# A fused attention, expert and MLP kernel: token rows in a DRAM region per expert, scattered in three rounds, and 32 idle matmuls between the loads of the branch codes

## Chip, cores and metric

The kernel runs on one core of one Trainium2 chip. The metric is the device time of one execution in microseconds (us), taken as the median of the runs. A profiled execution gives the trace; its times are counted from the start of its span.

## The reference, cut to what matters

Three layers in a row on 2 x 768 tokens of 384 values: a decayed linear attention, a layer that sends each token to one of eight experts, and a dense MLP with two matrices. The part that the change is about:

```python
x = attn_out.transpose(0, 2, 1, 3).reshape(B * S, H * D)      # token index = batch * 768 + position
logits = x @ w_gate                                           # 1536 x 8
expert_idx = np.argmax(logits, axis=1)
probs = softmax(logits); gate_w = probs[np.arange(N), expert_idx]
for i in range(N):                                            # the first `capacity` (384) tokens of an expert
    e = expert_idx[i]
    if counts[e] < capacity:
        disp[e, counts[e]] = x[i]; pos[i] = counts[e]; counts[e] += 1; keep[i] = True
y = np.einsum('ecf,efd->ecd', np.maximum(np.einsum('ecd,edf->ecf', disp, w1), 0.0), w2)
out[i] = gate_w[i] * y[expert_idx[i], pos[i]] if keep[i] else 0
h = out @ w_in
out = (np.maximum(h, 0) + alpha * np.minimum(h, 0)) @ w_out
```

## The kernel before, in words

Every f32 operand of the expert and MLP matmuls is split into a high and a low part (type fp32r), and a product is three matmuls: high x high, high x low, low x high (lines 1150 to 1152), or two where both parts of h are streamed at once (1160, 1161). ScalarE writes high parts, VectorE low parts.

The attention runs in three frames of 256 positions, each in eight steps of TensorE (`attend`, s = 2 to 9): transposes of q and k of a group, scores of the one before, and the product with v and the state of the one before that (`apply_group`, 1001). State tiles w0, w1, w2 are kept on VectorE's side; w0 starts as zeros and is first rewritten in `shift_state` (736 to 739) at step 8 of frame 0. A token tile has 128 tokens; there are twelve, by block of positions and batch. In the last frame the gate is worked in between: `x_transpose` (1041) turns a tile, ScalarE evicts it (483), `tile_logits` (1049) multiplies by w_gate; `LOGITS_AT` says which tiles go to which step.

After the last logits VectorE works on all twelve tiles at once (821 to 865): largest logit, one_hot of the chosen expert, gate weight. TensorE counts tokens per tile and expert (1128) and ranks them (1129 to 1133), so that VectorE gets one slot per token (`slots_i`), with the experts' tokens in one dense list of 1536. It raises `routed`, and then writes `base_i`: for each expert the first slot, plus 4096 (WIDE) if it has over 224 tokens (NARROW). GpSimd then issues twelve indirect scatters (369), which write each token's row of 388 values (384, gate weight and token number, two unused) to the DRAM tensor `rows_by_slot`. When all have landed, SyncE loads the list back as twelve tiles (308). TensorE turns each with three transposes of 128 x 128 (1144), ScalarE and VectorE write xs_hi and xs_lo (551, 877), which hold all 1536 tokens. Expert 0 starts when its tiles are there; `wait_ge(row_lo, rows)` asks for three tiles for expert 0 and for all twelve from expert 1 on.

An expert reads 224 columns of xs from its first slot (or 384 in the other branch), and has eight chunks of weights. Per chunk, `hidden(i)` makes 128 rows of h with nine matmuls, ScalarE and VectorE split h (561, 886), and `output(i)` adds to three PSUM banks with six matmuls. TensorE runs hidden two chunks ahead of output. Weights come by DMA from SyncE into a ring of eight buffers; ScalarE (543) and VectorE (870) split each six chunks ahead. The splits of chunks 0 to 5 stand ahead of the row tiles on both engines. TensorE reads the eight codes from base_i into registers (`value_load`, which the order of instructions shows as TENSOR_LOAD) before the transposes; ScalarE and VectorE read one ahead of each expert. In the profiled execution every expert took the branch of 224.

The order on each engine is the one written in the code; engines meet in semaphores only.

## Time and profile before

| | us |
|---|---|
| median of 3 runs (lowest, highest) | 549.45 (549.38, 549.66) |
| profiled execution | 548.02 |
| its span | 546.10 |
| TensorE matmuls busy | 467.5 (86%) |
| VectorE busy | 363.7 (67%) |
| ScalarE busy | 272.3 (50%) |
| GpSimd busy | 42.9 (8%) |
| mean granted clock of TensorE | 0.952 of full |

Busy time counts the engine's instructions, without register, branch and semaphore instructions. The granted clock is the share of full speed that TensorE was given; 0.50 is 1.2 GHz and 1.00 is 2.4 GHz. TensorE's load of weights has rows of its own (PEld) and runs beside the matmuls. A chain of waits names, from the end back, what each step waited for.

### The profile page before, as it was taken

Reading aid. Unit: us, or ns where it says so; the run is one execution under the profiler, and the core shown is the slowest. Engines: PE = TensorE matmul, PEld = TensorE weight load, DVE = VectorE, ACT = ScalarE, POOL = GpSimd, SP = SyncE. Lnnn points to the kernel's source line nnn. Section 1 sums busy time; section 2 is a strip of 40 time slices with the busy share of each in tenths; the row PEclk is TensorE's granted clock in tenths of the full one; section 3 lists DMA queues with packets and bytes.
Section 4 is the critical chain, followed back from the end, with each engine's and each line's share of the span. In section 5 each row is a group of like instructions: output and inputs, shape, how many; then the busy total and the mean of one; then the engine's idle time right before and its main releaser. Section 6 shows DMA issues by size and latency. Waiting matters only on the chain.

```text
span 546.1 us, 10002 instructions
## 1 busy us (share of the span) xinstructions
PE 467.5 (86%) x3752; PEld 417.7 (76%) x3752; DVE 363.7 (67%) x624; ACT 272.3 (50%) x431; POOL 42.9 (8%) x48
## 2 busy tenths in 40 slices
PE   0538976999996029999999999999999999999995
PEld 0237755777885029999999998989998899889985
DVE  2688798678534317776777776778747787487751
ACT  5996758673446017666666664433334333334212
POOL 2000000000001890000000000000002000110002
PEclk9959999999998559999999999999999999999999
DMA  8970000000000469667666666233324333230001
GB/s 323 424 294 2 3 1 1 2 1 2 2 3 2 159 188 324 182 192 215 205 195 199 200 189 190 89 99 104 96 78 145 102 101 114 70 108 0 1 0 60
DMA packets 22178, 63.69 MB, mean 117 GB/s; under 512 B 2928, under 2 KB 4464, under 8 KB 22128
## 3 DMA queue, kind: packets, MB, share of 16 engines
q1 hardware_dynamic: 20592, 58.27, 32.6%
q0 software_dynamic: 1536, 4.74, 2.3%
q8 instruction: 32, 0.52, 0.4%
q14 instruction: 18, 0.15, 0.1%
HBM read 58.27 MB, written 4.74 MB: 115 GB/s over the span
## 4 chain that ended last, share of the span: by engine, by line
PE 74%; DVE 8%; DMA 5%; issue 5%; POOL 3%; ACT 2%; SPq 2%; DVEq 0%; POOLq 0%; ACTq 0%
PE banks L1152 15%; PE banks L1150 15%; PE banks L1151 15%; PE banks L1160 7%; DMA vv<-v_rows 4%; PE banks L1161 3%; PE banks L998 3%; POOL rows_by_slot L369 3%; PE banks L986 2%; PE banks L1017 2%; PE banks L989 2%; PE banks L950 2%; PE banks L1020 1%; PE banks L1144 1%; PE banks L1046 1%
## 5 line engine op out<-in xcount | busy, mean ns | idle before, releaser
L870 DVE TENSOR_TENSOR w_lo<-raw_early,w_hi 128x768 fp32r<-128x768 f32 x84 | 80.0, 956 | 31.1 <-ACT w_hi L543 30.0
L588 ACT ACTIVATE g_hi<-g_all 128x512 fp32r<-128x512 f32 x48 | 30.3, 632 | 118.4 <-DVE g_all L923 118.4
L543 ACT ACTIVATE w_hi<-raw_early 128x768 fp32r<-128x768 f32 x84 | 70.4, 843 | 33.2 <-PE banks L1161 32.7
L1150 PE MATMUL banks<-w_hi,g_hi 128*128 128x384 f32 x192 | 65.1, 339 | 0.5 <-DVE g_lo L925 0.5
L1152 PE MATMUL banks<-w_hi,g_lo 128*128 128x384 f32 x192 | 65.0, 339 | 0.0
L1151 PE MATMUL banks<-w_lo,g_hi 128*128 128x384 f32 x192 | 64.9, 338 | 0.0
L1160 PE MATMUL banks<-h_hi_lo,w_hi 128*128 128x448 f32 x192 | 64.0, 378 | 0.9 <-DVE h_hi_lo L886 0.9
L925 DVE TENSOR_TENSOR g_lo<-g_all,g_hi 128x512 fp32r<-128x512 f32 x48 | 33.3, 693 | 44.2 <-ACT g_hi L588 44.2
L1150 PE MATMUL banks<-ys_hi,w_hi 128*128 128x512 f32 x144 | 56.1, 390 | 1.2 <-DVE ys_lo L900 1.2
L1152 PE MATMUL banks<-ys_hi,w_lo 128*128 128x512 f32 x144 | 57.1, 397 | 0.0
L1151 PE MATMUL banks<-ys_lo,w_hi 128*128 128x512 f32 x144 | 56.8, 394 | 0.0
L1150 PE MATMUL banks<-xs_hi,w_hi 128*128 x192 | 52.7, 274 | 0.1
L1151 PE MATMUL banks<-xs_lo,w_hi 128*128 x192 | 52.6, 274 | 0.0
L1152 PE MATMUL banks<-xs_hi,w_lo 128*128 x192 | 52.6, 274 | 0.0
L1161 PE MATMUL banks<-h_hi_lo,w_lo 128*128 128x224 f32 x192 | 50.9, 265 | 0.0
L921 DVE TENSOR_SCALAR g_neg<-banks,alpha 128x512 f32<-128x512 f32 x48 | 35.8, 746 | 7.5 <-PE banks L1152 7.4
L1160 PEld LDWEIGHTS banks<-h_hi_lo,w_hi 128*128 128x128 f32 x192 | 36.2, 189 | 4.4 <-DVE h_hi_lo L886 2.1
L1150 PEld LDWEIGHTS banks<-w_hi,g_hi 128*128 128x128 f32 x192 | 36.1, 188 | 3.4 <-DVE g_lo L925 1.5
L1151 PEld LDWEIGHTS banks<-w_lo,g_hi 128*128 128x128 f32 x192 | 36.1, 188 | 2.1
L1150 PEld LDWEIGHTS banks<-xs_hi,w_hi 128*128 128x128 f32 x192 | 36.7, 191 | 1.1 <-issue 0.4
L377 POOL DMA_INDIRECT out_rows<-xq,tok_slot x12 | 11.9, 991 | 324.5 <-ACT xq L597 322.7
L1152 PEld LDWEIGHTS banks<-xs_hi,w_lo 128*128 128x128 f32 x192 | 36.9, 192 | 0.0
(166 smaller groups left out, 981.2 us busy)
## 6 DMA issues: line engine op xcount, KB each, us to landing
raw_early<-weights SPq DMA_DIRECT2D x84, 384.0 KB, 3.5
raw_late<-weights SPq DMA_DIRECT2D x28, 384.0 KB, 3.5
xq<-q_rows SPq DMA_DIRECT2D x3, 776.0 KB, 16.6
xq<-rows_by_slot SPq DMA_DIRECT2D x12, 194.0 KB, 4.5
kk<-k_rows SPq DMA_DIRECT2D x3, 768.0 KB, 18.0
vv<-v_rows SPq DMA_DIRECT2D x3, 768.0 KB, 19.4
aa<-a_re_rows SPq DMA_DIRECT2D x2, 768.0 KB, 10.5
th<-a_im_rows SPq DMA_DIRECT2D x2, 768.0 KB, 11.9
```

What stands on the lines that cost most here:

```text
L369: pool.indirect_dma_start(xs_dram, bass.IndirectOffsetOnAxis(ap=slots_i[:, t:t + 1], axis=0), xq[:, x:x + XW], None).then_inc(scattered, 16)
L543: A(wh[:, slot, :], raw[slot], ACT.Copy).then_inc(w_hi, 1)
L588: A(gh[:, c % GBUF, :], gg[:, c % GBUF, :], ACT.Copy).then_inc(g_hi, 1)
L870: TT(wl[:, slot, :], raw[slot], wh[:, slot, :].bitcast(F32), ALU.subtract).then_inc(w_lo, 1)
L921: TS(gn[:, :], HM[c % HBUF][:, :], 0.0, alpha[:, i:i + 1], ALU.min, ALU.mult).then_inc(g_neg, 1)
L925: TT(gl[:, c % GBUF, :], gg[:, c % GBUF, :], gh[:, c % GBUF, :].bitcast(F32), ALU.subtract).then_inc(g_lo, 1)
L998: x = MM(SC[g % 2][:, c], lhsT=kT[:, g % 2, c], rhs=qT[:, g % 4, c], start=True, stop=True)
L1150: MM(o, lhsT=whi, rhs=mhi, start=first, stop=False)
L1151: MM(o, lhsT=whi, rhs=mlo, start=False, stop=False)
L1152: return MM(o, lhsT=wlo, rhs=mhi, start=False, stop=last)
L1160: MM(both, lhsT=whi, rhs=hs[:, slot, :, 0:n], start=first, stop=False)
L1161: return MM(o[:, 0:n], lhsT=wlo, rhs=hh[:, slot, 0:n], start=False, stop=last)
```

## The change

**Regions.** `rows_by_slot` becomes `rows_by_expert`: 8 regions of 1536 rows of 384 values. In a region, tokens of batch 0 are laid downward from its middle and those of batch 1 upward, so that a token's row depends only on earlier tiles of its own batch. Rows around each middle (768) are first set to zero by eight DMAs out of w0, behind the input loads; GpSimd's first scatter and VectorE's first write of w0 wait for them. An expert's tokens are a window of 384 rows that starts at `start_i`; SyncE reads that start into a register and loads the window.

**Rounds.** Tiles 0 to 7, 8 and 9, 10 and 11 are routed one round after another: `choose(r)` and `place(r)` on VectorE, `rank(r)` on TensorE. Rounds 0 and 1 stand within the last frame's steps 5 to 8. The transposes and logits of the gate are dealt out anew to its steps (up to three tiles in one).

**Windows.** xs_hi and xs_lo hold two windows instead of all tokens. Only the two tiles of expert 0's window are turned ahead of expert 0; those of expert e + 1 are turned within expert e, behind output 1 and 4 on TensorE and at chunks 3 and 6 on the others. The third tile of a window is turned in the branch of 384 alone. Loads of window e + 2 are queued on SyncE ahead of the chunks of expert e.

**Gate weight and token number** leave the row and go by a second set of twelve scatters (8 bytes a token) to `meta_by_slot`, which SyncE loads at expert 4. What VectorE computes for them stands in pieces (`gate_part`) within expert 0.

**Codes.** The branch code needs the count alone (`wide_i`, semaphore `flags`), and ahead of each of TensorE's eight register loads stand four f32 matmuls of ones and ident whose result nobody reads.

**Outputs** of the experts rotate over four PSUM banks instead of five.

```diff
-        LOGITS_AT = {2: (0, 1), 3: (2, 3), 4: (4, 5), 5: (6, 7), 6: (8,), 8: (9,), 9: (10,), 10: (11,)}
+        X_IN = {2: ((0,), (1,), (2,)), 3: ((3,), (4,), (5,)), 4: ((6,), (7,), ()), 5: ((), (), (8,)),
+                7: ((9,), (), ()), 8: ((), (), (10,)), 10: ((11,), (), ())}
+        LOGITS_IN = {2: ((), (0,), (1,)), 3: ((2,), (3,), (4,)), 4: ((5,), (6,), (7,)),
+                     6: ((), (), (8,)), 7: ((), (9,), ()), 9: ((10,), (), ())}
...
+            sp.wait_ge(consts, 1)
+            for e in range(E):
+                sp.dma_start(xs_dram[e * REGION + MID - CAP:e * REGION + MID + CAP, :].rearrange(
+                    "(p t) w -> p t w", t=ZT), w0[0:2 * CAP // ZT, None, 0:UW].to_broadcast([2 * CAP // ZT, ZT, UW])
+                    ).then_inc(zeroed, 16)
...
+            sp.wait_ge(scattered, 16 * NT)
+            for t in range(WT):
+                sp.dma_start(win[:, 0, t, :], window_rows(start_rows[0], t, 1)[:, 0, :]).then_inc(first_dma[t], 16)
...
-            pool.wait_ge(routed, 1)
-            for t in range(NT):
...
+            pool.wait_ge(zeroed, 16 * E)
+            for r, (n0, n1) in enumerate(ROUNDS):
+                pool.wait_ge(routed, r + 1)
+                for t in range(B * n0, B * n1):
+                    pool.indirect_dma_start(xs_dram, bass.IndirectOffsetOnAxis(ap=slots_i[:, t:t + 1], axis=0),
+                                            xq[:, t * UW:(t + 1) * UW], None).then_inc(scattered, 16)
...
+            act.wait_ge(logits_made, XT_FREE + NT)
+            for i in range(FIRST):
+                split_hi(i, i, 1)
...
+            for t in range(NTILES):
+                window_hi(0, t)
+            for i in range(FIRST, AHEAD):
+                split_hi(i, i, 1)
...
+                    if nxt is None and s == 5:
+                        choose(0)
+                    if nxt is None and s == 6:
+                        place(0)
...
+                        if s == 7:
+                            choose(1)
+                        if s == 8:
+                            place(1)
...
+            choose(2)
+            place(2)
...
+            TS(wide_i[0:1, :], count[0:1, :], float(NARROW), float(WIDE), ALU.is_gt, ALU.mult).then_inc(flags, 1)
...
+                        if e == 0:
+                            gate_part(i)
+                        if i in NEXT_AT and e + 1 < E:
+                            window_lo(e + 1, NEXT_AT.index(i))
...
+            def rank(r):
...
+                MM(to, lhsT=ones[:, :], rhs=before[:, n0:n1, :, :].rearrange("p n b e -> p (n b e)"), start=True, stop=False)
+                pe.wait_ge(onehot, r + 1)
+                MM(to, lhsT=upto[:, :], rhs=one_hot[:, B * n0:B * n1, :].rearrange("p t e -> p (t e)"),
+                   start=False, stop=True).then_inc(ranked, 1)
...
+            pe.wait_ge(flags, 1)
+            codes = []
+            for e in range(E):
+                for _ in range(WARM):
+                    MM(bank[0][:, 0:P], lhsT=ident[:, :], rhs=ones[:, :], start=True, stop=True)
+                codes.append(pe.value_load(wide_i[0:1, e:e + 1], min_val=0, max_val=WIDE))
+            for t in range(NTILES):
+                window_T(0, t)
...
+                        if i in NEXT_FROM and e + 1 < E:
+                            window_T(e + 1, NEXT_FROM.index(i))
```

TensorE, from the last logits to expert 0, before (L1129 to L1133 are the ranks, L1138 the code loads, L1144 the transposes of all twelve tiles):

```order
L1129 MATMUL banks<-one_hot,after 128x96
L1131 MATMUL banks<-upto,tile_counts 128x96
L1133 MATMUL banks<-upto,tile_counts 128x8
L1138 TENSOR_LOAD base_i
L1138 ISA x2
...
L1144 MATMUL banks<-ident,xq 128x128 x36
L1204 COMPARE_AND_BRANCH
```

The same place now (L1234 and L1236 are rank(2), L1310 the ends of the regions, L1331 the idle matmuls, L1319 the transposes):

```order
L1234 MATMUL banks<-before,ones 128x16
L1236 MATMUL banks<-one_hot,upto 128x16
L1310 MATMUL banks<-before,ones 128x16
L1331 MATMUL banks<-ones,ident 128x128 x4
L1332 TENSOR_LOAD wide_i
L1332 ISA x2
...
L1319 MATMUL banks<-ident,xq 128x128 x6
L1393 COMPARE_AND_BRANCH
```

Matmuls and load alternate eight times; 30 of 36 transposes are gone from here, and two groups of three stand in each of the experts 0 to 6 instead.

VectorE, the first chunks of expert 0 (L1042 is the low half of h, L875 the split of weights, the others the first parts of the gate), where before L886 and L870 alternated with nothing between:

```order
L1042 SCALAR_TENSOR_TENSOR h_hi_lo<-banks,h_hi_lo 128x224
L875 TENSOR_TENSOR w_lo<-raw_late,w_hi 128x768
L1004 TENSOR_TENSOR slot_less_start<-prefix_steps,window_start 128x8
L999 TENSOR_TENSOR route<-slot_less_start,one_hot 128x96
L1006 TENSOR_REDUCE route_small<-route 128x12
L1042 SCALAR_TENSOR_TENSOR h_hi_lo<-banks,h_hi_lo 128x224
L875 TENSOR_TENSOR w_lo<-raw_late,w_hi 128x768
L999 TENSOR_TENSOR route<-window_start,one_hot 128x96
L1009 TENSOR_REDUCE route_small<-route 128x12
L1010 TENSOR_TENSOR route_small<-route_small 128x12
```

Twenty such instructions come in between, and the low halves of two tiles of the next window (L879).

## Rows read from the trace of the kernel before

**Rows 1.** The page's slices: TensorE's busy tenths and its granted clock, 40 slices.
```profile
PE   0538976999996029999999999999999999999995
PEclk9959999999998559999999999999999999999999
```

**Rows 2.** Chain of waits, 168 to 215 us: start us, us, what.
```profile
170.99 0.55 PE banks L1054 x12
...
173.55 0.48 PE banks L1128 x2
...
176.98 0.19 DVE xq L860
...
177.45 1.11 POOL rows_by_slot L369
...
195.42 2.58 DMA rows_by_slot<-xq,slots_i
...
208.82 0.37 PE banks L1150
```

**Rows 3.** Timeline of VectorE's routing: start us, us, engine, line, operation, out<-in.
```profile
172.60 0.26 DVE L834 TENSOR_TENSOR route<-route,prior 128x96 f32<-128x96 f32 x1
...
172.89 0.25 DVE L835 TENSOR_REDUCE route_small<-route 128x12 f32<-128x96 f32 x1
...
177.26 0.17 DVE L864 TENSOR_SCALAR many_more<-many_more 128x8 f32<-128x8 f32 x1
```

**Rows 4.** Timeline at the scatters; last a window: stretch, length, busy by engine.
```profile
177.58 5.28 DVE L870 TENSOR_TENSOR w_lo<-raw_early,w_hi 128x768 fp32r<-128x768 f32 x6
...
178.87 4.83 POOL L369 DMA_INDIRECT rows_by_slot<-xq,slots_i  x1 [0.30 <-issue]
184.01 0.96 POOL L369 DMA_INDIRECT rows_by_slot<-xq,slots_i  x1 [0.30 <-issue]
...
160.00:170.00 10.00, 9.73 (x198) 8.70 (x196) 1.41 (x3) 3.54 (x7) 0.14 (x1) 1.00 0.01 3
```

The window's columns, here and in rows 8: length, then busy us and count of PE, PEld, DVE, ACT, POOL, then the granted clock, the DMA share and GB/s.

**Rows 5.** Timeline at the load of the tiles: first transposes and low halves.
```profile
200.48 1.54 PE L1144 MATMUL banks<-ident,xq 128*128 128x128 f32 x6 [25.05 <-DMA xq<-rows_by_slot]
...
201.95 1.20 DVE L877 TENSOR_TENSOR xs_lo<-banks,xs_hi 128x384 fp32r<-128x384 f32 x2 [19.09 <-ACT xs_hi L551]
```

**Rows 6.** Chain of waits: groups of transposes and of f32 matmuls on TensorE.
```profile
39.70 1.71 PE banks L998 x8
...
42.91 0.89 PE banks L998 x8
...
145.71 0.48 PE banks L1046 x3
146.19 0.44 PE banks L986 x4
```

**Rows 7.** Windows of TensorE: stretch, length, busy, granted clock, DMA share, GB/s.
```profile
172.00:173.00 1.00, 0.00 (x0) 0.64 0.00 0
...
188.00:192.00 4.00, 0.00 (x0) 0.50 0.43 164
...
206.00:207.00 1.00, 1.00 (x9) 0.80 1.08 387
...
208.00:209.00 1.00, 0.85 (x6) 1.00 1.03 409
```

**Rows 8.** Windows of two experts, the first and the last, all engines.
```profile
208.80:224.50 15.70, 15.68 (x120) 15.31 (x121) 10.90 (x19) 9.90 (x18) 0.00 (x0) 1.00 0.80 258
...
320.40:336.50 16.10, 16.09 (x122) 15.30 (x120) 12.05 (x23) 10.47 (x21) 0.00 (x0) 1.00 0.67 201
```

**Rows 9.** Timeline of VectorE at the start of expert 1.
```profile
227.29 0.39 DVE L886 SCALAR_TENSOR_TENSOR h_hi_lo<-banks,h_hi_lo 128x224 fp32r<-128x224 f32 x1 [0.62 <-issue]
227.59 0.95 DVE L870 TENSOR_TENSOR w_lo<-raw_late,w_hi 128x768 fp32r<-128x768 f32 x1
```

**Rows 10.** Chain of waits: VectorE's first work on w0 beyond reading it.
```profile
80.70 0.56 DVE wtmp L736
```

More of the change, by code:

```diff
@@ L43, in fused_attention_moe_mlp @@
     DP = SINE + D
-    XW = UW + 4
     G4 = 4
@@ L94, in fused_attention_moe_mlp @@
         prior = sb("prior", [P, E])
+        sign = sb("sign", [P, B, E])
+        low = sb("lowest_start", [P, E])
         logit = sb("logit", [P, NT, E])
+        one_hot = sb("one_hot", [P, NT, E])
+        before = sb("before", [P, NB + 1, B, E])
+        rt = sb("route", [P, 3, NT, E])
+        rs = sb("route_small", [P, 10, NT])
+        ends = sb("region_ends", [P, B, E])
+        start = sb("window_start", [P, E])
+        steps_of = sb("prefix_steps", [P, 4, PADE + E])
+        count, first = steps_of[:, 0, PADE:PADE + E], steps_of[:, 3, PADE - 1:PADE - 1 + E]
+        move = sb("slot_less_start", [P, E])
+        wide_f = sb("wide", [P, E])
         slots_i = sb("slots_i", [P, NT], I32)
+        comp_i = sb("compact_i", [P, NT], I32)
+        start_i = sb("start_i", [1, E], I32)
+        wide_i = sb("wide_i", [1, E], I32)
         base_i = sb("base_i", [1, E], I32)
+        meta_src = sb("meta_src", [P, NT, 2])
+        meta = sb("meta", [P, NT, 2])
         tok_slot = sb("tok_slot", [P, NT], I32)
@@ L855, in _ @@
-            dve.tensor_reduce(slot, rt[:, 3, :, :], AX_X, ALU.add)
-            then(dve.tensor_reduce(start, rt[:, 4, :, :], AX_X, ALU.add))
-            TS(slots_i[:, :], slot, -1.0, None, ALU.add)
-            then(STT(keep, slot, -float(CAP), start, ALU.add, ALU.is_le))
-            TT(xcols[:, :, :, DM], gate.rearrange("p (b n) -> p b n", b=B), keep.rearrange("p (b n) -> p b n", b=B),
-               ALU.mult).then_inc(routed, 1)
-            then(TT(many_more[:, :], ends, first[:, :], ALU.subtract))
@@ new lines, in _ @@
+            for i in range(3):
+                then(TT(steps_of[:, i + 1, PADE:PADE + E], steps_of[:, i, PADE:PADE + E],
+                        steps_of[:, i, PADE - (1 << i):PADE + E - (1 << i)], ALU.add))
+            TT(base_i[0:1, :], first[0:1, :], wide_f[0:1, :], ALU.add).then_inc(bases, 1)
+            dve.tensor_copy(logit[:, B * (NB - 1):NT, :], LB[:, B * (NB - 1) * E:NT * E].rearrange("p (t e) -> p t e", e=E)
+                            ).then_inc(logits_out, 1)
+            TT(start[:, :], ends[:, 0, :], low[:, :], ALU.max)
@@ L1130, in _ @@
[L1130 to L1146 removed]
+            x_transpose(NT - 1)
@@ new lines, in _, with tile_T @@
+            tile_logits(NT - 1)
+            rank(2)
+            pe.wait_ge(prefixed, NB)
+            MM(ENDS[:, 0:B * E].rearrange("p (b e) -> p b e", b=B), lhsT=ones[:, :], rhs=before[:, NB, :, :],
+               start=True, stop=True).then_inc(summed, 1)
+            def tile_T(e, t):
+                if e == 0:
+                    pe.wait_ge(first_dma[t], 16)
+                elif t == 0:
+                    pe.wait_ge(win_dma[e], 16)
+                for k in range(KB):
+                    x = pe.transpose(turned_rows(e, t)[:, k * P:(k + 1) * P], win[:, e % WB, t, k * P:(k + 1) * P], ident[:, :])
+                return x
```

406 lines of the change are left out of this document (250 added, 156 removed).

## Prediction

> **What bounds the kernel now.** I read the page first for its slices, and the reader is to see one hole in them: TensorE stands at 9 tenths before and after it, at 0 in it, and its granted clock reads 5 there [rows 1]. Then the chain of waits in order of time, from the end of the attention to the first expert matmul [rows 2]: the last gate logits end at 171.54 us, VectorE and TensorE choose experts and count slots until 177.17, GpSimd issues the indirect scatters from 177.45, the last lands at 198.0 (195.42 + 2.58), and expert 0's first matmul starts at 208.82. So 37.3 us lie between the last logits and the experts. Last the sums by stretch [rows 8]: an expert takes 15.7 to 16.1 us with TensorE busy for nearly all of it and VectorE for 10.9 to 12.1. What is taken out of the hole is gained; what is put on TensorE in the experts is paid in full.
>
> **The parts, in the clock of the profiled span.**
>
> *Start.* GpSimd sets up more constants before it releases the others, eight short instructions at 0.1 to 0.2 us. Behind that the first DMAs land anyway; I put 0.3 us on the path (0 to 1).
>
> *Attention.* The twelve transposes and logits of the gate are moved between steps, not added; but tile 10's logits (at 0.55 us, as the last tile's) [rows 2] now stand ahead of the last apply group, where before they ran under ScalarE's eviction. New are rank(0) and rank(1), four f32 matmuls of two passes each: an estimate of 0.45 and 0.35 us, from the two passes of L1128 at half clock, 0.48 us [rows 2]. Three tiles a step instead of two make TensorE wait for ScalarE's evictions: I put 0.9 us (0 to 2.5). The last logits end at 171.54 + 0.55 + 0.45 + 0.35 + 0.9 = 173.8.
>
> *Last round of the routing.* choose(2) handles two tiles. A dependent VectorE instruction on 96 elements comes every 0.29 us, 0.26 and a gap of 0.03; one on 8 or 12 elements lasts 0.17, so 0.2 [rows 3]. Five of the latter and the pair that writes one_hot are 1.2 us; the rank matmul until VectorE can read it 0.5, as L1128 took; the three instructions of place(2) 0.65. `routed` reaches 3 at 173.8 + 2.35 = 176.2. Before, this part took 5.6 us [rows 2], now 2.4. The flag per expert follows 0.8 later, at 177.0.
>
> *Scatters.* Each costs GpSimd 0.96 + 0.30 us [rows 4]. Eight are released by place(0), near 161.3, two by place(1), two by the last round. Eight take 10.1 us and end near 171.5, the next two at 174; the last starts at 176.2 + 0.28 + 1.27 = 177.7 and lands 2.58 later, at 180.3, against 198.0. From there to the first transposed tile the trace has 2.46 us (198.02 to 200.48) [rows 2, 5]: 182.8. One row stands out: the second scatter took 4.83 us, and beside it VectorE ran six splits of weights, 177.58 to 182.86, without a pause [rows 4]; it ended 0.84 us, about one scatter, after them. Early scatters run beside VectorE as well, but VectorE is busy for only 1.41 of the 10 us from 160 to 170 [rows 4], and the path below leaves 6.5 us of slack, so I charge nothing.
> The Trainium skill (GPSIMD Engine Reference, Key points) says that GpSimd shares its SBUF interfaces with VectorE and contends with VectorE instructions that have two SBUF inputs; the splits are such instructions, and by that rule the trace agrees. By it the sum stays as it is while the early scatters are held for less than the slack; held each as long as that one they give the last rival.
>
> *The idle matmuls become the bound.* At 177.0 TensorE starts 32 f32 matmuls of 128 columns, two passes each, 64 in all, with eight register loads between. A pass takes 0.214 us at half clock (8 in 1.71) and 0.111 at full (8 in 0.89) [rows 6]. The clock fell to 0.50 within 172 to 173, once TensorE's dense work had ended at 169; after dense work began again at 37.8 it rose between 41.4 and 42.9, where equal rows halve [rows 6], after that of 203.0 within 206 to 207 [rows 7]. So the idle matmuls begin at half, and I take the rise after 4.0 us. No row shows a register load. Near it: VectorE, between two experts, did one load and a branch in a gap of 0.62 us with nothing else to wait for [rows 9]. Bounds are 0 (the load runs while matmuls are queued) and 0.62; I take 0.45, since both loads and matmuls stand in one engine's order and the gap holds a branch too. Two groups at half: 2 x (8 x 0.214 + 0.45) = 4.3; six at full: 6 x (8 x 0.111 + 0.45) = 8.0. TensorE is free at 189.3, 6.5 us after the rows are there.
>
> *To the first expert matmul.* Only two tiles are transposed first, not twelve. From the first transpose to the end of the second tile's low half the trace has 200.48 to 203.15, 2.7 us at half clock [rows 5]; 2.5 at full. Expert 0 starts at 191.8, against 208.8: 17.0 us gained.
>
> *Experts.* Other work that the hole hid now stands here.
> (a) Seven experts carry six transposes for the next one. Three cost 0.33 us by L986 (four in 0.44) and 0.48 by L1046 [rows 6]; I take 0.8 per expert (0.67 to 0.96).
> (b) Expert 0: VectorE has three splits (2.6), load and branch (0.6), then eight pairs of low half and split (8 x 1.34 = 10.7) [rows 9], two low halves of the next window (1.2) [rows 5] and 20 instructions of the gate, seven on 96 elements (2.0) and thirteen small ones (2.6). That is 19.7 us; less the last split 18.7, when the last output chunk may start (0.95 more). Expert 0 then takes 19.7 instead of 15.7, +4.0, transposes included.
> (c) Experts 1 to 6: 0.8 each, and 0.2 for a low half that comes later behind the window's tile: +6.0. Expert 7: nothing. Sum +10.0 (6 to 14). The trace's 1.1 us that a split waits for ScalarE at times stays hidden.
> Weights: SyncE now issues a window and eight chunks at each expert's start. At the 409 GB/s of 208 to 209 [rows 7] 3.7 MB take 9 us of 17; covered. The gate's 12 small scatters and GpSimd's memsets end long before the MLP. Nothing of the MLP changes.
>
> *Zeroing* moves 8 x 768 rows of 1,536 B, 9.4 MB, from about 37.5, when the loads end, and VectorE may write w0 at 80.70 only behind it [rows 10]. At 409 GB/s, at which weights and the last rows of almost this length were read near 208, it takes 23 us and is hidden. The trace shows no such write; the scatters wrote at 164 GB/s [rows 7], but at GpSimd's pace. Bounds: 0 and 14 us on the path; I take 0, since the SyncE queue does not have that pace.
>
> **Sum.** -17.0 + 10.0 + 0.3 = -6.7 us. Span 546.1 becomes 539.4; the profiled run (548.02, 1.92 around its span) 541.3. The median of the runs is 549.45, 1.43 above that, so 542.7.
>
> **Rivals.**
> *Loads ride under the matmuls.* They cost nothing: TensorE is free at 177.0 + 4.0 + (64 - 19) x 0.111 = 186.0, 3.3 us earlier: 539.4. For it: matmuls are issued ahead of their ends. Against it: VectorE's gap.
> *The clock stays at half through the idle matmuls*, since a fifth of their time is gaps. Eight groups take 17.3 us, 5.0 more, and transposes and 3.4 us of expert matmuls at half cost 2.0: 549.7, no change. For it: both rises in the trace came after denser work. Against: 200.5 to 206 was sparse at first too.
> *The experts cost their upper bound*, VectorE being late in every one by some 0.9 us: +5, 547.7. Against: it has 4 us to spare in 16 [rows 8] and gets 1.2 of work.
> *Slower: the zeroing is late.* Its deadline is 43 us after its start, a rate of 218 GB/s. At 164 GB/s it ends at 95, VectorE waits 14 us in frame 0 and TensorE with it: 557. It decides from 218 GB/s down.
> *Slower: the scatters don't run early*, since VectorE holds GpSimd. With 4.83 + 0.30 us for each of the eight, the last lands some 31 us later than I have it, at 211, and the experts start at 216: 567. It decides from 6.5 us of delay on; VectorE's load in that stretch bears it out poorly.
>
> **How the numbers follow.** Forecast 0.50 (539.8 to 546.5), loads under matmuls 0.20, half clock 0.11, dear experts 0.09, late zeroing 0.07, late scatters 0.03. A measurement of this kernel can tell 0.2%, 1.1 us, from no change. Faster: forecast, hidden loads, dear experts, 0.79. Same: most of half clock, 0.10. Slower: the last two and a dearer half clock, 0.11. The range goes from the hidden loads with cheap experts (539.4 less 3) to the half-clock case: 536 to 550.
>
> **What would show it.** A row of the last scatter near 180 and a first transpose near 189 whose wait is not for the DMA; the granted clock at 0.50 from 174 and 1.00 from 181; expert 0 at 19 to 20 us with TensorE waiting for the low half, the next six at 17.0; VectorE at w0 with no wait for the zeroing. I am wrong if the first transposes wait for the DMA of the window, if the clock is still at 0.50 when expert 0 starts, or if experts 1 to 6 are over 17.5 us.

## The result, and the profile after

The changed kernel took **554.74 us** (median of 4 runs, 553.93 to 555.55) beside 549.56 for the kernel before: a ratio of 1.0101, 95% interval 1.0086 to 1.0116, so 5.2 us slower. The forecast was 542.7, faster, and its range ended at 550. The profiled run took 555.55 us, with a span of 553.8.

Where the time stands, in the clock of each span:

| | before | forecast | after |
|---|---|---|---|
| last gate logits end | 171.5 | 173.8 | 185.8 |
| first transposes for expert 0 | 200.5 | 189.3 | 198.3 |
| expert 0's first matmul | 208.8 | 191.8 | 200.5 |
| expert 0, expert 1 (us) | 15.7, 15.9 | 19.7, 17.0 | 18.0, 24.7 |
| experts 2 to 6, mean (us) | 16.0 | 17.0 | 16.8 |
| first matmul of the MLP | 337.7 | 330.7 | 344.9 |

So 12.0 us were lost against the forecast before the last logits, 3.3 of them were made good until expert 0 began and 1.7 in it, and 7.7 were lost again in expert 1. The page's slices answer to [rows 1]: the hole has not gone, it is shallower and longer.

```profile
PE   0538976999986799799999999999999999999995
PEclk9959999999996599899999999999999999999999
```

The first loss, in the timeline of ScalarE, VectorE, TensorE and GpSimd (start us, us, engine, line, operation, then in brackets the idle time ahead of it and what ended that):

```profile
160.85 0.69 DVE L790 TENSOR_TENSOR scores<-banks,upto 128x512 f32<-128x512 f32 x1
171.75 0.69 DVE L790 TENSOR_TENSOR scores<-banks,upto 128x512 f32<-128x512 f32 x1 [10.21 <-remote]
...
167.48 0.60 ACT L531 ACTIVATE qT<-banks 112x512 f32<-112x512 f32 x1 [6.06 <-remote]
...
163.39 0.60 PE L1153 MATMUL banks<-ident,k_rot 128*112 128x128 f32 x4
...
164.15 1.06 PE L1162 MATMUL banks<-qT,kT 112*128 112x128 f32 x8
169.45 0.71 PE L1222 MATMUL banks<-wgate,xT 128*64 128x8 f32 x12 [4.24 <-issue]
...
161.79 1.11 POOL L424 DMA_INDIRECT rows_by_expert<-xq,slots_i  x1 [156.56 <-DVE slots_i L869]
163.21 0.96 POOL L424 DMA_INDIRECT rows_by_expert<-xq,slots_i  x1 [0.30 <-issue]
...
170.80 0.96 POOL L424 DMA_INDIRECT rows_by_expert<-xq,slots_i  x1 [0.30 <-issue]
```

The transposes L1153 stand as over at 163.99, and ScalarE, which needs nothing else, takes their result at 167.48. The scores L1162 stand as over at 165.21, and VectorE takes them at 171.75. Six of its updates are late beside the eight early scatters, and one more, by 1.1 us at 181.8, beside the next two. The scatters themselves ran at their 0.96 + 0.30 us. That is the hole in the reading of [rows 4]: I looked at what delays GpSimd, and not at what GpSimd delays. The pause then let the clock fall, and the rest of the attention ran at half of it (window: length, busy us of PE, PEld, DVE, ACT, POOL, granted clock, DMA share, GB/s):

```profile
164.00:168.00 4.00, 1.21 (x11) 1.02 (x9) 0.00 (x0) 0.52 (x2) 3.04 (x4) 1.00 0.42 152
168.00:172.00 4.00, 2.17 (x34) 2.04 (x35) 0.25 (x1) 1.05 (x3) 2.88 (x3) 0.70 0.40 148
172.00:176.00 4.00, 3.29 (x25) 2.74 (x25) 1.94 (x10) 0.49 (x1) 0.00 (x0) 0.50 0.13 49
```

The second loss is of the same kind. GpSimd issues the twelve small scatters of gate and token number from 215.7 to 231.9, and in expert 1 TensorE's matmuls come one by one, 0.7 us apart, and the others wait for them (the granted clock falls again as well, to 0.50 in the window from 232 to 236):

```profile
230.73 0.26 PE L1338 MATMUL banks<-xs_hi,w_hi 128*128 128x224 f32 x1 [0.94 <-issue]
231.45 0.55 PE L1339 MATMUL banks<-xs_lo,w_hi 128*128 128x224 f32 x1 [0.45 <-issue]
232.16 0.35 PE L1340 MATMUL banks<-xs_hi,w_lo 128*128 128x224 f32 x1 [0.16 <-issue]
...
233.57 0.36 ACT L629 ACTIVATE h_hi_lo<-banks 128x224 fp32r<-128x224 f32 x1 [4.77 <-remote]
```

Between the two, the idle matmuls, the answer to [rows 6] and [rows 5]:

```profile
188.89 9.60 PE L1331 MATMUL banks<-ones,ident 128*128 128x128 f32 x64 [0.79 <-DVE wide_i L974]
198.33 0.82 PE L1319 MATMUL banks<-ident,xq 128*128 128x128 f32 x6
200.46 0.37 PE L1338 MATMUL banks<-xs_hi,w_hi 128*128 128x224 f32 x1 [1.31 <-DVE xs_lo L879]
```

### The profile page after: what moved, and what is told of

It reads as the page before. It is cut to its first block, busy times and chain, and to the rows that moved or that the text cites. A ratio compares the mean times of both kernels' runs of the same rounds, so it can differ in the third digit from the quotient of the medians.

```text
span 553.8 us, 10070 instructions
## 1 busy us (share of the span) xinstructions
PE 486.7 (88%) x3834; PEld 435.0 (79%) x3834; DVE 371.6 (67%) x671; ACT 270.2 (49%) x435; POOL 50.4 (9%) x64
## 4 chain that ended last, share of the span: by engine, by line
PE 66%; DVE 11%; DMA 7%; issue 6%; ACT 3%; SPq 3%; another core or an unknown queue 1%; DVEq 1%; POOL 0%; ACTq 0%; POOLq 0%
PE banks L1340 14%; PE banks L1338 14%; PE banks L1339 14%; PE banks L1348 6%; DMA vv<-v_rows 4%; DMA raw_early<-weights 3%; PE banks L1162 3%; PE banks L1349 3%; PE banks L1181 2%; PE banks L1150 2%; PE banks L1184 2%; PE banks L1153 2%; PE banks L1114 2%; PE banks L1222 1%
## 5 line engine op out<-in xcount | busy, mean ns | idle before, releaser
L875 DVE TENSOR_TENSOR w_lo<-raw_early,w_hi 128x768 fp32r<-128x768 f32 x84 | 80.0, 956 | 27.7 <-ACT w_hi L602 23.7
L1348 PE MATMUL banks<-h_hi_lo,w_hi 128*128 128x448 f32 x192 | 65.7, 386 | 2.9 <-DVE h_hi_lo L1042 2.6
L1338 PE MATMUL banks<-xs_hi,w_hi 128*128 128x224 f32 x192 | 54.3, 283 | 2.6 <-DVE xs_lo L879 1.3
L1339 PE MATMUL banks<-xs_lo,w_hi 128*128 128x224 f32 x192 | 53.5, 279 | 1.5 <-issue 1.5
L1340 PE MATMUL banks<-xs_hi,w_lo 128*128 128x224 f32 x192 | 53.2, 277 | 0.2 <-issue 0.2
L1339 PEld LDWEIGHTS banks<-xs_lo,w_hi 128*128 128x128 f32 x192 | 37.4, 195 | 3.1 <-issue 3.1
L1349 PEld LDWEIGHTS banks<-h_hi_lo,w_lo 128*128 128x128 f32 x192 | 37.1, 193 | 0.8 <-issue 0.8
## 6 DMA issues: line engine op xcount, KB each, us to landing
xq<-q_rows SPq DMA_DIRECT2D x3, 768.0 KB, 16.6
kk<-k_rows SPq DMA_DIRECT2D x3, 768.0 KB, 17.9
vv<-v_rows SPq DMA_DIRECT2D x3, 768.0 KB, 19.2
```

What stands on the lines that cost most here:

```text
L875: TT(wl[:, slot, :], raw[slot], wh[:, slot, :].bitcast(F32), ALU.subtract).then_inc(w_lo, 1)
L1338: MM(o, lhsT=whi, rhs=mhi, start=first, stop=False)
L1339: MM(o, lhsT=whi, rhs=mlo, start=False, stop=False)
L1340: return MM(o, lhsT=wlo, rhs=mhi, start=False, stop=last)
L1348: MM(both, lhsT=whi, rhs=hs[:, slot, :, 0:n], start=first, stop=False)
L1349: return MM(o[:, 0:n], lhsT=wlo, rhs=hh[:, slot, 0:n], start=False, stop=last)
```

## The experiments

Runs that were sent together ran on one chip beside the kernel before, and that turned out to matter: the kernel before took 548.7 to 549.8 us on every chip, the changed one did not. I call them A (the result above) and B to F; B to F are five different chips, and A may be one of the last three. Theory 1 was that scatters in a row stall the other engines; the rivals were the routing rounds themselves (theory 2) and the plain work of the experts (theory 4).

### Chip B: each burst taken out of the way

`late`: all row scatters wait for the last round. `meta_plain`: a plain store in token order in place of the small scatters, so that gates and output rows come out wrong; it serves for its time alone. `late_meta_plain`: both. `no_warm`: no idle matmuls.

```diff
             pool.wait_ge(zeroed, 16 * E)
+            pool.wait_ge(routed, len(ROUNDS))
             for r, (n0, n1) in enumerate(ROUNDS):
...
-            for t in range(NT):
-                pool.indirect_dma_start(meta_dram, ...).then_inc(meta_scattered, 16)
...
-                    sp.wait_ge(meta_scattered, 16 * NT)
+                    sp.wait_ge(meta_ready, 1)
+                    sp.dma_start(meta_dram.rearrange("(t p) w -> p t w", p=P), meta_src[:, :, :]).then_inc(meta_scattered, 16)
+                    sp.wait_ge(meta_scattered, 16)
...
-    WARM = 4
+    WARM = 0
```

> Change: the eight row scatters of the first round wait, like the others, until the last round of routing is done; nothing else is moved. Theory 1 (a burst of GpSimd scatters while the attention runs stalls ScalarE, VectorE and TensorE there, and the pause lets TensorE's clock fall): ScalarE's wait of 6.06 us and VectorE's of 10.21 us after 161 us are gone, the granted clock stays 1.00 to the last logits, and these end at 172 to 175 us of the span instead of 185.8. Theory 2 (the routing rounds themselves, the waits for the ranks and three tiles in a step, are what makes the attention long): the last logits stay at 182 us or later. The twelve scatters then end some 15 us after the last slots, so that expert 0 starts about 16 us after its earlier place relative to the logits: by theory 1 the kernel's time is 548 to 554, by theory 2 560 to 566.

> Change: the twelve indirect scatters of gate and token number that GpSimd issues in expert 1 are left out, and one plain store of SyncE in token order takes their place (so the rows go out with the wrong gates and to other rows of the output: this part of the computation is changed). Theory 1 (the scatters stall the other engines while they are issued): expert 1 takes 16.5 to 17.2 us from first matmul to first matmul like experts 2 to 6, in place of some 19.5, its granted clock stays 1.00, and the kernel is 2.5 to 4 us faster than the changed kernel (550.5 to 552.5). Theory 4 (expert 1 is long for its instructions, the last transposes and splits): no change, 554 to 556.

> Change: both of the above: all row scatters after the last round of routing, and gate and token number stored plainly in token order by SyncE (so gates and output rows are changed). Theory 1: both gains add, last logits at 172 to 175 us and expert 1 of 17 us, time 2.5 to 4 us below that of the kernel with the late scatters alone (545 to 551). If instead the stalls come from something else, the time is 558 to 566.

> Change: none of the idle matmuls between the loads of the branch codes; the eight loads stay. The codes were through at 198.3 us while the last row scatter landed at 192.4 and the first window followed some 2.5 us later, so without the matmuls the windows bind: if the loads and the windows alone count, the first transposes stand at 195 to 196 us instead of 198.3 and the kernel gains 2 to 3 us. Against that stands the clock, which was at half until 193 us: if the idle matmuls were what raised it, expert 0 starts at half clock and loses 2 to 5 us, so that the kernel is 0 to 3 us slower than the changed kernel (555 to 558). If transposes and expert 0's own matmuls raise it at once: 551.5 to 553.

| chip B | us | ratio to before, 95% | last logits | expert 0 starts | experts 0, 1 |
|---|---|---|---|---|---|
| late | 554.50 | 1.0071 to 1.0122 | 175.2 | 201.1 | 20.5, 21.2 |
| meta_plain | 536.45 | 0.975 to 0.9787 | 174.7 | 190.0 | 17.6, 17.0 |
| late_meta_plain | 549.23 | 0.999 to 1.0027 | 174.1 | 200.1 | 20.1, 17.0 |
| no_warm | 538.47 | 0.9787 to 0.9826 | 175.0 | 186.9 | 20.2, 19.7 |

`late` alone fits theory 1, but the others break it as it was put: `meta_plain` and `no_warm` scatter eight tiles in the attention just as the changed kernel does, and their last logits end at 175. Both came out 13 to 14 us below the ranges expected for them. Two numbers can be read on this chip all the same. The early scatters are worth 12.8 us (549.23 less 536.45); 10.1 of them lie ahead of expert 0, and 2.5 in it, where `late_meta_plain` begins at half clock. And expert 1 takes 17.0 us without the small scatters and 19.7 to 21.2 with them, though no update of TensorE is late: `late` and `late_meta_plain` differ in them alone, and ScalarE's waits for weights from 185 to 245 sum to 12.0 and 8.9 us. That late weights are the whole of it was not tested.

### Chip C: is it the kernel or the chip?

`after_again` is the changed kernel, unedited. `phase` lets the first scatter wait for `masked` as well, 0.8 us. `warm2` has `WARM = 2`. `paced_meta_no_warm` has `WARM = 0`, and `pool.wait_ge(used, USED_FREE + RING + 2 * t + 1)` ahead of each small scatter.

> The changed kernel once more, with nothing edited, beside the three that follow on one chip. It is here because the two kernels without the idle matmuls and without the scatters of expert 1 both ran some 16 to 18 us faster than the changed kernel, and in both the last logits ended at 175 us instead of 185.8 with the same early scatters. If the long attention belongs to the kernel: 554 to 556 us, last logits at 184 to 187. If it belonged to the chip or the hour: 541 to 546, last logits at 174 to 176.

> Change: the first of the early scatters also waits until VectorE has masked the next scores, which moves the burst about 0.8 us later against the attention's work; nothing is added to or taken from the engines' work. Theory A (TensorE is starved while scatters are issued, and whether it is hangs on how the burst meets a moment of the attention): last logits at 174 to 176, time 542 to 546. Theory B (it hangs on how TensorE's program lies, which idle matmuls and weight of code shift): no change, 554 to 556, since GpSimd's one added wait leaves TensorE's program alone.

> Change: two idle matmuls ahead of each branch code in place of four. Theory B (the layout of TensorE's program decides whether the attention stalls): last logits either near 175 or near 185, not between. If the attention is fast here: the codes take 5 to 7 us, first transposes bound by the windows or the codes at 184 to 186 us, kernel 538 to 542. If the attention is slow: 550 to 554.

> Change: no idle matmuls, and the twelve scatters of gate and token number are issued one for every second chunk of experts 1 to 3 (each waits for TensorE's count of used chunks) instead of all in a row. Theory 1 (a burst stalls the engines, single scatters do not): expert 1 takes 17.0 us as with the plain store instead of 19.7, expert 0 17.6 to 18.5 instead of 20.2, kernel 533 to 536. If every scatter costs the same wherever it stands: the 5 us come back in experts 1 to 3, kernel 537 to 539.

| chip C | us | ratio to before, 95% | last logits | first transposes | experts 0 to 4 |
|---|---|---|---|---|---|
| after_again | 537.96 | 0.9768 to 0.98 | 174.3 | 187.5 | 17.6, 17.9, 17.3, 16.9, 16.6 |
| phase | 538.26 | 0.9774 to 0.9807 | 175.0 | 186.8 | 18.2, 19.2, 16.7, 16.9, 16.6 |
| warm2 | 536.96 | 0.9752 to 0.9788 | 174.3 | 183.9 | 19.9, 18.4, 16.7, 16.9, 16.6 |
| paced_meta_no_warm | 541.09 | 0.9826 to 0.9859 | 173.9 | 183.0 | 20.0, 17.0, 17.8, 18.2, 19.0 |

**The same kernel is 11.8 us faster than the one before on C and 5.2 us slower on A.** The rows that stood apart on A stand together on C:

```profile
163.43 0.60 PE L1153 MATMUL banks<-ident,k_rot 128*112 128x128 f32 x4
...
164.20 1.06 PE L1162 MATMUL banks<-qT,kT 112*128 112x128 f32 x8
...
164.07 0.60 ACT L531 ACTIVATE qT<-banks 112x512 f32<-112x512 f32 x1 [2.61 <-PE banks L1153]
...
165.29 0.69 DVE L790 TENSOR_TENSOR scores<-banks,upto 128x512 f32<-128x512 f32 x1 [3.71 <-PE banks L1162]
...
164.00:168.00 4.00, 3.67 (x64) 3.39 (x62) 2.10 (x9) 1.96 (x4) 3.09 (x4) 1.00 0.43 157
```

ScalarE follows L1153 at 164.07 beside four scatters in the same 4 us (POOL 3.09). TensorE is busy for 3.67 of them, against 1.21 on A. The difference of 17.9 us until the MLP is the two stretches: 11.5 to the last logits, 0.6 less to expert 0's start, 0.4 in expert 0, 6.8 in expert 1, and 0.2 less behind it.

None of the four kernels fell in a range expected for it; the first three were 1 to 4 us faster. And as nothing holds TensorE on C, `phase` and `warm2` say nothing on whether the moment of the burst or the layout of TensorE's program matters where it is held.

The idle matmuls: with two a code the transposes come 3.6 us earlier, but expert 0 grows from 17.6 to 19.9 us, since its weights are then late; 1.0 us remains. Without any, the clock is where the forecast feared it, in `no_warm` and in `warm2` from 182 us:

```profile
182.00:186.00 4.00, 1.54 (x6) 1.07 (x6) 0.35 (x1) 0.73 (x2) 4.00 (x2) 0.50 0.76 191
186.00:190.00 4.00, 3.10 (x14) 3.10 (x15) 3.70 (x6) 3.26 (x6) 3.74 (x1) 0.50 0.95 313
```

```profile
182.00:186.00 4.00, 2.69 (x20) 2.46 (x18) 1.02 (x2) 1.62 (x4) 4.00 (x2) 0.84 0.92 220
186.00:190.00 4.00, 4.00 (x32) 3.85 (x33) 3.94 (x6) 3.78 (x7) 3.04 (x1) 1.00 0.99 361
```

Yet the half clock costs little there: expert 0 takes 20.2 us in `no_warm` and 19.9 in `warm2`. As far as two chips can be compared, the idle matmuls are worth little: 538.47 us without any on B, 536.96 with two a code and 537.96 with four on C.

`paced_meta_no_warm` is a miss (541.1 us, 533 to 536 expected): expert 1 is at 17.0, but expert 0 stayed at 20.0, the last scatter started at 258, and SyncE's wait for it stood ahead of weights, so that the DMA queues stood nearly idle from 256 to 264 (share 0.16) and expert 4 took 19.0. Spacing work out moves its end, and whoever waits for the end must be able to.

### Chip D: the changed kernel again, and two attempts to mend it

`mlp_meta`: two idle matmuls a code; the small scatters wait for the last expert, and GpSimd loads the result itself, while ScalarE's and VectorE's waits for it stand within the MLP. `mlp_meta_late_first`: also four weight chunks issued earlier. `no_next`: the changed kernel, in which TensorE skips the transposes of the next window, so that later experts compute on wrong rows; it ran once.

```diff
             pool.wait_ge(meta_ready, 1)
+            pool.wait_ge(used, USED_FREE + RING * E)
             for t in range(NT):
                 pool.indirect_dma_start(meta_dram, ...).then_inc(meta_scattered, 16)
+            pool.wait_ge(meta_scattered, 16 * NT)
+            pool.dma_start(meta[:, :, :], meta_dram.rearrange("(t p) w -> p t w", p=P)).then_inc(meta_dma, 16)
...
+            for i in range(AHEAD, RING):
+                sp.dma_start(raw[i], w_in[i, :, :]).then_inc(w_dma[i], 16)
             sp.wait_ge(scattered, 16 * NT)
...
-                            window_T(e + 1, NEXT_FROM.index(i))
+                            pe.wait_ge(row_lo, NTILES * (e + 1) + NEXT_FROM.index(i))
+                            pe.sem_inc(row_T, 1)
```

> The changed kernel with nothing edited, for the third time. It took 554.7 us where it was first compared and 538.0 on another chip; the kernel before took 549.3 to 549.8 on every chip so far. If the first comparison's late TensorE (its semaphore updates came up to 6.5 us late at 161 to 173 us of the span and up to 7 us late at 224 to 234) is a property of a few chips: 537 to 539 on most. If it comes and goes on any chip: 537 to 556, and runs of one call would spread.

> Change: two idle matmuls ahead of each branch code (as in the kernel of 537.0 us), and the twelve scatters of gate and token number wait until all experts are done; GpSimd itself waits for their landing and loads them back, so SyncE's queue of weights is free of that wait. Theory 1 (the scatters of expert 1 delay the weights and stretch experts 0 and 1): expert 1 takes 17.0 us instead of 18.4, the matmuls of the MLP start 1.4 us earlier and lose nothing to the scatters, kernel 534.5 to 536. If scatters cost the same beside the MLP: 536.5 to 538.

> Change: as the kernel with the scatters in the MLP, and the four weight chunks that were issued behind the first window are issued ahead of the wait for the last row scatter, at about 178 us instead of 184. Expert 0 took 19.9 us when it began at 186.0 and 17.6 when it began at 189.6, and ScalarE waited there for weights, so by the reading that transfers bound its end, 4 us of transfers moved ahead of the windows shorten expert 0 to 17 us: kernel 531.5 to 533.5. If the four transfers only delay the last scatters and the windows: first transposes 1 to 3 us later, kernel 534 to 537.

> Change: TensorE leaves out the transposes of the next expert's rows in experts 0 to 6 (six passes each), while ScalarE and VectorE still copy and split as before; the experts after the first compute on wrong rows. Forecast: the transposes cost 0.8 us of each expert, so experts 2 to 6 take 15.9 to 16.2 us, as in the kernel before, instead of 16.6 to 16.9, and the kernel is 4.5 to 5.5 us faster than the changed kernel. If what stretches the experts is ScalarE's and VectorE's extra work: under 2 us.

| chip D | us | last logits | first transposes | experts 0, 1 | MLP starts | MLP to end |
|---|---|---|---|---|---|---|
| after_c3 | 553.73 | 185.5 | 198.1 | 17.6, 24.9 | 343.9 | 208.1 |
| mlp_meta | 547.65 | 186.3 | 195.6 | 19.9, 17.0 | 336.0 | 209.8 |
| mlp_meta_late_first | 546.26 | 186.3 | 196.1 | 18.2, 17.0 | 334.9 | 209.5 |
| no_next | 555.13 | 187.0 | 200.0 | 17.6, 24.9 | 344.7 | 208.7 |

D behaves as A: all four kernels have last logits between 185.5 and 187.0, and the latest update in their attention is 5.1 or 6.5 us late. It goes with the chip, then, and comes back there almost unchanged; it isn't noise. Moved to the MLP the twelve small scatters cost 1.1 to 1.7 us there (209.8 less the 208.7 or 208.1 of the two kernels without them) instead of the 7.9 of expert 1; TensorE's updates are late again, by up to 4.0 us, but only from 344.5 on, nine us behind the first scatter. The four chunks shorten expert 0 by 1.7 us, to 18.2 where 17 was expected, and the first transposes come 0.5 us later; `mlp_meta_late_first` is 1.4 us faster where 3 were expected. The absolute times expected are missed by 12 us, because of the chip. `no_next` missed: experts 2 to 6 sum to 82.5 us in place of 83.6, so the six transposes are worth some 0.2 us per expert and not 0.8. That ScalarE's and VectorE's copies make up the rest was only argued.

### Chip E: what it is in the scatters

The kernel before issues its twelve scatters in a row too, 1.26 us apart [rows 4], but beside a TensorE that stands idle (0.00 us busy from 188 to 192 [rows 7]). So its like times on every chip don't speak against the scatters, and a burst can be put where TensorE works. `spaced`: each early scatter waits for the landing of the one before. `before_burst`: the kernel before, with eight scatters added that nobody reads. `before_plain`: the same blocks by plain DMAs. The last two ran once each.

```diff
                 for t in range(B * n0, B * n1):
+                    if r == 0 and t > 0:
+                        pool.wait_ge(scattered, 16 * t)
...
+            pool.wait_ge(masked, SC_FREE + 8 * (NF - 1) + 6)
+            for t in range(8):
+                pool.indirect_dma_start(burst, bass.IndirectOffsetOnAxis(ap=burst_i[:, t:t + 1], axis=0),
+                                        upto[:, :], None).then_inc(burst_out, 16)
...
+            sp.wait_ge(masked, SC_FREE + 8 * (NF - 1) + 6)
+            for t in range(8):
+                sp.dma_start(burst[t * P:(t + 1) * P, :], upto[:, :]).then_inc(burst_out, 16)
```

> Change: each of the eight early row scatters waits until the one before it has landed (some 2.7 us apart instead of 1.26); the twelve scatters in a row of expert 1 stay as they are and tell which kind of chip this is: expert 1 of 24.7 us where TensorE is held, 17.9 to 21 where it is not. Theory C (what holds TensorE is how thick the scatters come): on a chip that holds it, the last logits end at 175 to 178 us instead of 185.5 to 187, and the scatters of the first round end at about 183. Theory D (any scatter in flight holds it): last logits at 184 us or later. On a chip that does not hold it: 174 to 176 either way.

> The kernel before with one thing added: eight indirect scatters of 128 rows of 512 B from a constant tile to an extra DRAM tensor, in a row, when VectorE has masked the sixth group of scores of the last frame (160 us); nobody reads them. Theory 1 (a row of scatters on GpSimd is enough to hold TensorE, none of the other edits is needed): on a chip that holds it the last logits end 9 to 12 us later than 171.5 us; on the others at 171.5 to 172.5. Theory 2 (the three tiles a step, the rank matmuls or the rows' reading are needed): within 1 us of 171.5 also where the changed kernel is held.

> The kernel before with the same eight blocks of 128 rows of 512 B written at the same moment, but by eight plain DMAs that SyncE issues. Theory 1a (GpSimd's making of descriptors and the semaphore traffic of its scatters hold TensorE, not the writing): last logits at 171.5 to 172.5 on every chip. Theory 1b (any burst of small DMA writes does it): 9 to 12 us later where the scatters do that.

| chip E | us | last logits | TensorE's updates in the attention late by at most |
|---|---|---|---|
| spaced | 553.12 | 175.7 | 0.7 us |
| before_burst | 556.81 | 180.5 | 6.5 us |
| before_plain | 548.70 | 172.6 | none over 0.3 |

The old kernel with nothing but eight scatters added loses 7.6 us (the kernel before has 549.23 on this chip), and its rows are those of A. Timeline of `before_burst`, and the windows of `before_burst` and `before_plain`:

```profile
160.72 1.12 POOL L367 DMA_INDIRECT burst<-upto,burst_rows  x1 [155.87 <-DVE scores L725]
...
169.72 0.96 POOL L367 DMA_INDIRECT burst<-upto,burst_rows  x1 [0.30 <-issue]
...
170.73 0.69 DVE L725 TENSOR_TENSOR scores<-banks,upto 128x512 f32<-128x512 f32 x1 [10.30 <-remote]
...
164.00:168.00 4.00, 1.93 (x27) 1.13 (x26) 0.00 (x0) 1.08 (x2) 3.09 (x4) 1.00 0.15 50
168.00:172.00 4.00, 1.47 (x13) 0.98 (x11) 0.69 (x1) 0.00 (x0) 2.07 (x3) 0.66 0.15 49
```

```profile
164.00:168.00 4.00, 4.00 (x73) 3.66 (x74) 1.38 (x2) 1.50 (x4) 0.00 (x0) 1.00 0.20 58
168.00:172.00 4.00, 3.21 (x80) 2.69 (x76) 0.00 (x0) 1.46 (x3) 1.05 (x2) 1.00 0.01 4
```

Same bytes, same moment, 58 GB/s against 50: with plain DMAs TensorE is busy for all of the 4 us. So it is not the writing (1b falls), and none of the other edits is needed (2 falls). What remains is GpSimd's issuing (1a); its making of descriptors and its semaphores weren't told apart. And the rate decides: in `spaced` the scatters start 2.8 to 3.5 us apart, each in the attention still takes its 0.96, and TensorE is late by 0.7 us at most. There expert 1, with its twelve in a row, still takes 23.9, and its updates come up to 8.0 us late.

### Chip F: the remedy

Both kernels have the small scatters beside the MLP, each behind the landing of the one before, the four chunks earlier and `WARM = 2`. They differ in how the early scatters are drawn apart, `paced_fills` by the first piece, `paced_landed` by the second:

```diff
                 for t in range(B * n0, B * n1):
+                    if r == 0 and t > 0:
+                        for _ in range(3):
+                            then(pool.memset(meta[:, :, :], 0.0))
...
+                    if 0 < t < 5:
+                        pool.wait_ge(scattered, 16 * t)
```

> The changed kernel with nothing edited, once more, so that the two repaired kernels stand beside it on one chip: 553.5 to 555.5 us where TensorE is held, 537.5 to 538.5 where it is not.

> Changes: the eight early scatters are drawn apart to about 2.1 us each by three small fills on GpSimd ahead of each (1.26 us apart before); the scatters of gate and token number stand beside the MLP and each waits for the landing of the one before; four weight chunks are issued ahead of the wait for the last row scatter; two idle matmuls a code. Theory C (the rate of the scatters decides): last logits at 174 to 176 us on every chip, no late updates of TensorE in the experts, kernel 535 to 538 on both kinds of chip. If a rate of one in 2.1 us is still too thick: last logits at 177 to 183 where TensorE is held, kernel 538 to 544 there.

> Changes: as the kernel with the fills, but the first five early scatters are drawn apart by the wait for the landing of the one before (2.9 us apart), and the rest come in a row. The five end at about 174.5 us, the row behind them when the last logits are nearly through. Theory C: last logits at 174.5 to 177 us on every chip, last scatter at about 183, kernel 536 to 540 on both kinds.

| chip F | us | ratio to before, 95% | last logits | expert 0 starts | experts 0, 1 |
|---|---|---|---|---|---|
| after_c5 | 555.29 | 1.0088 to 1.0131 | 186.4 | 201.4 | 17.6, 25.0 |
| paced_fills | **538.00** | 0.9788 to 0.9821 | 175.7 | 190.0 | 18.8, 17.0 |
| paced_landed | 540.07 | 0.9825 to 0.9858 | 175.3 | 192.4 | 18.9, 17.0 |

F holds TensorE, and there `paced_fills` beats the changed kernel by 17.3 us and the one before by 10.9. Of the 17.3, the last logits show 10.7, which only the spacing of the early scatters explains; the rest comes from the other three edits together. Its scatters and the stretch beside them:

```profile
162.77 1.12 POOL L424 DMA_INDIRECT rows_by_expert<-xq,slots_i  x1 [157.53 <-DVE slots_i L873]
164.66 0.97 POOL L424 DMA_INDIRECT rows_by_expert<-xq,slots_i  x1 [0.28 <-POOL meta L423]
...
175.05 0.97 POOL L424 DMA_INDIRECT rows_by_expert<-xq,slots_i  x1 [0.28 <-POOL meta L423]
...
164.00:168.00 4.00, 3.67 (x64) 3.42 (x63) 1.49 (x6) 1.47 (x3) 2.95 (x11) 1.00 0.31 113
168.00:172.00 4.00, 3.25 (x57) 2.98 (x57) 1.80 (x8) 0.98 (x2) 3.09 (x9) 1.00 0.38 141
```

The three fills gave a spacing of 1.73 us, not 2.1, and it was enough: no update of TensorE over 0.55 us late, and 3.67 us busy of 4 as on C. `paced_landed` ended 0.07 us above the range expected for it. In both the granted clock is back near 0.50 from 188 on and still there when expert 0 begins (0.54 and 0.50 in the window from 188 to 192), so they don't reach what this order could give. Neither ran on a chip like B or C.

## Why the forecast was wrong

Mechanism by mechanism, on A and on C, where nothing held TensorE:

- **Scatters.** The step that failed is "so I charge nothing", said of early scatters beside working engines. It weighed one direction, VectorE holding GpSimd, and found slack for it. The cost came the other way, GpSimd's scatters holding TensorE, and on a path without slack: 11.5 us to the last logits (A against C) and 6.8 in expert 1, where "The gate's 12 small scatters and GpSimd's memsets end long before the MLP" looked at their end alone. On C, where TensorE isn't held, the small scatters still have a price that was left out: expert 1 takes 17.9 us with them there, and 17.0 without them on B. The Trainium skill (GPSIMD Engine Reference, Key points) had led me to VectorE's splits; here a scatter and a split with two SBUF inputs ran side by side at 189.8, and neither was longer:

```profile
189.83 0.96 POOL L424 DMA_INDIRECT rows_by_expert<-xq,slots_i  x1 [0.30 <-issue]
...
189.86 2.70 DVE L875 TENSOR_TENSOR w_lo<-raw_early,w_hi 128x768 fp32r<-128x768 f32 x3
```

  So the trace agrees with that rule less than I wrote. The second scatter's 4.83 us came back as 4.97 in `before_burst`, at its usual place behind the routing, and stays unexplained.
- **Slower by late scatters (0.03)** was the rival that named the right engine with the wrong victim. None of the rivals was what happened; those on the slower side had 567 and 557.
- **Attention** otherwise: 173.8 forecast, 174.3 on C. The two ranks, the moved tile and the stalls were sized well in their sum; no run tells them apart. 185.8 on A is the burst and the half clock behind it.
- **Last round:** 2.35 us from the logits to `routed` forecast; 185.79 to 188.29, 2.5, measured. **Last scatter** at 178.4 on C, 177.7 forecast; at 189.8 on A, late like all behind the logits.
- **Codes.** Forecast 12.3 us from the flags to the transposes. Measured 9.4 on A and 10.1 on C. The 64 passes start 0.213 us apart until 193.5 on A and 0.112 apart from there, the values of [rows 6], and only the first is followed by more (0.37): no gap stands at any of the eight loads. The loads ride under the matmuls; the rival of 0.20 was right, and the 3.6 us charged for them (8 x 0.45) were not there. The 0.45 was taken from [rows 9], a gap of VectorE's that had a branch in it. The codes still bound expert 0 where there were four matmuls a code; with two, the windows did, at 183.9.
- **Clock.** "1.00 from 181" came at 183.3 on C (0.58 in the window from 180 to 184, 1.00 in the next): right in kind, but the idle matmuls had run for 5.9 us and not 4.0. On A it was at 0.50 from 170 on, and they brought it back at 193.5, after 4.6.
- **Experts.** +10.0 forecast, +8.5 on C (137.4 in place of 128.9). Expert 0 took 17.6 to 18.0, not 19.7: the twenty gate instructions fit beside it. What bounds it hangs on the last row scatter, behind which its window and four chunks are loaded: in all 14 profiles with that order expert 0 ends 27.4 to 28.9 us behind that scatter's start, whether it took 17.6 us or 20.5, so that it is long where it begins early. Experts 1 to 6 at 17.0: 16.6 and 16.9 in turn from the third on, right in size; but the reason, six transposes of 0.8, did not bear the test (0.2 by `no_next`). The prediction's own sign of being wrong, an expert over 17.5 us, came in expert 1: 24.7 on A and 17.9 on C.
- **Zeroing.** Hidden: the transfers end at 66 us, at 300 to 400 GB/s and then less, and VectorE's first work on the state behind it comes at 81.30 without a wait, [rows 10] shifted by the 0.6 us of the later start.

With the steps as they came out on C, the gains are 19.2 to expert 0's start, less 8.5 in the experts and 0.4 in the MLP: 10.3 of span, 535.8 us, where I had 539.4. The forecast would have been 4.7 us too slow there, inside its range, and nearer to the rival of the hidden loads (539.4 for 538.0 measured). On A its span was 14.4 us too short: 18.0 for the one cost that it had set to nothing, less 3.6 by which the rest was too dear.

## What to carry to other kernels

Ask of work moved beside a busy engine not only whether that engine delays it, but whether it delays the engine, and put a price on it even where no row shows one: here, on some chips and in runs that were all recorded, a row of indirect scatters every 1.26 us cost up to 11.5 us, and one every 1.73 us next to nothing. Draw a row of scatters apart, or put it where TensorE has little in flight, and look that no queue waits for its end. And have the changed kernel timed on a second chip before its cause is argued: the kernel before agreed within 0.2% wherever it ran, the changed one took 538.0 us on C and 553.7 to 555.3 on A, D and F.

## What had not been expected of the hardware

- Of five different chips, three (D, E, F; and A, which may be one of them) hold TensorE while GpSimd issues scatters 1.26 us apart; its semaphore updates come up to 6.5 us late in the attention and 8.0 in expert 1. On B and C no update is over 0.3 us late under the same scatters.
- How soon it begins differs: with the first scatter in the attention, five to nine us in for expert 1, nine for the MLP. TensorE issues some 60, 30 and 20 matmuls in 4 us there, so a backlog that fills with its instructions would fit; this was not tested.
- On the chips that hold TensorE, records of the trace are missing too: those of A and D have 2580 to 2660 of 2976 landings of DMA queues, the traces of C at least 2945. They are missing there also where nothing is held: `before_plain` on E lacks 89 of 2800, `paced_fills` on F 190 of 2976. So a chip on which the recording keeps up less well is a rival that no run here rules out: the recording may itself be part of what holds TensorE. Every run here was recorded, and the same kernels without it would decide.
- Eight register loads of TensorE cost nothing between queued matmuls: the passes around them start 0.213 us apart at half clock and 0.112 at full, without a gap.
